# Channel mixers of an attention–mixer kernel by one level of Strassen (Winograd's seven products), on one core

## The reference, cut to what matters

```
q_s = exp(q - max_d q) / (sum_d + 1e-9);  k_s = exp(k - max_s k) / (sum_s + 1e-9)
x   = q_s @ (k_s^T v)                        # per batch and head, heads side by side: 576 x 512
u   = x + (relu(x^T w_tok1) w_tok2)^T        # token mixer, 576 -> 256 -> 576
y   = u + relu(u @ w_ch1) @ w_ch2            # stage B: 512 -> 1536 -> 512 (w1b, w2b)
yn  = (y - mean) / sqrt(var + 1e-6) * g_ln
out = y + relu(yn @ w1c) @ w2c               # stage C: 512 -> 2048 -> 512
```

## Time and profile before

| | |
|---|---|
| median of three runs | 1640.64 us |
| span of the profiled execution, its own time | 1637.3 us |
| TensorE busy (matmul) | 1611.0 us, 98% |
| VectorE busy | 600.8 us, 37% |
| ScalarE busy | 357.4 us, 22% |
| GpSimd busy | 242.7 us, 15% |
| moved by DMA | 120.17 MB, 73 GB/s over the span |

### The profile page before, as it was taken

How to read it: one execution, slowest core, us unless ns; L and a number is a source line. 1 busy time by engine, 2 the same in 40 slices (tenths; PEclk the granted TensorE clock), 3 DMA queues, 4 the chain that set the end, 5 groups by cost and what they waited for, 6 DMA issues and landing times.

```text
span 1637.3 us, 20140 instructions
## 1 busy us (share of the span) xinstructions
PE 1611.0 (98%) x7748; PEld 1354.0 (83%) x7748; DVE 600.8 (37%) x940; ACT 357.4 (22%) x643; POOL 242.7 (15%) x211
## 2 busy tenths in 40 slices
PE   6999999999999999999989999999999999999999
PEld 5899998888888888888868888888888888888887
DVE  7878751212212212122362424333333333342411
ACT  4556551111111111111221111111121111111110
POOL 5565658000000000000840000000000000000000
PEclk9999999999999999999999999999999999999999
DMA  7777744202102022021330200102020202020100
GB/s 245 244 225 233 226 153 154 93 1 77 54 23 77 0 77 77 0 77 64 104 116 1 70 8 19 58 0 77 0 77 0 77 0 77 0 77 0 51 0 27
DMA packets 72883, 120.17 MB, mean 73 GB/s; under 512 B 4944, under 2 KB 23952, under 8 KB 72848
## 3 DMA queue, kind: packets, MB, share of 16 engines
q1 hardware_dynamic: 68368, 105.01, 19.5%
q0 software_dynamic: 4480, 14.68, 2.8%
HBM read 91.36 MB, written 28.31 MB: 73 GB/s over the span
## 4 chain that ended last, share of the span: by engine, by line
PE 96%; DVE 2%; DMA 1%; SPq 0%; ACT 0%; issue 0%; DVEq 0%
PE bank L844 30%; PE bank L846 30%; PE bank L845 30%; PE bank L868 3%; PE bank L879 1%; PE bank L959 1%; PE bank L901 1%; PE bank L900 1%; DVE x_in L803 1%; DMA vt<-v 0%; DMA qt<-q 0%; PE bank L990 0%; PE bank L991 0%; PE bank L853 0%; DVE ln L792 0%
## 5 line engine op out<-in xcount | busy, mean ns | idle before, releaser
L809 DVE SCALAR_TENSOR_TENSOR h_lo<-bank,h_hi 128x512 fp32r<-128x512 f32 x252 | 174.1, 691 | 951.7 <-ACT h_hi L569 951.7
L569 ACT ACTIVATE h_hi<-bank 128x512 fp32r<-128x512 f32 x252 | 151.0, 599 | 1134.5 <-PE bank L846 1134.5
L846 PE MATMUL bank<-x_hi,w_early 128*128 128x512 f32 x576 | 224.1, 389 | 0.0
L845 PE MATMUL bank<-x_lo,w_early 128*128 128x512 f32 x576 | 224.1, 389 | 0.0
L844 PE MATMUL bank<-h_hi,w_early 128*128 128x512 f32 x576 | 224.1, 389 | 0.0
L845 PE MATMUL bank<-h_lo,w_early 128*128 128x512 f32 x576 | 224.1, 389 | 0.0
L846 PE MATMUL bank<-h_hi,w_early 128*128 128x512 f32 x576 | 224.1, 389 | 0.0
L844 PE MATMUL bank<-x_hi,w_early 128*128 128x512 f32 x576 | 224.1, 389 | 0.0
L844 PE MATMUL bank<-x_hi,w_late 128*128 128x512 f32 x432 | 168.8, 391 | 7.2 <-DVE x_lo L753 7.2
L845 PE MATMUL bank<-x_lo,w_late 128*128 128x512 f32 x432 | 168.5, 390 | 0.0
L846 PE MATMUL bank<-x_hi,w_late 128*128 128x512 f32 x432 | 168.5, 390 | 0.0
(11 more groups left out here) (113 smaller groups left out, 1925.8 us busy)
## 6 DMA issues: line engine op xcount, KB each, us to landing
kt<-kT SPq DMA_DIRECT2D x32, 288.0 KB, 5.7
u_scratch<-u_out SPq DMA_DIRECT2D x32, 288.0 KB, 2.7
x_in<-u_scratch SPq DMA_DIRECT2D x9, 1024.0 KB, 6.8
res<-u_scratch SPq DMA_DIRECT2D x9, 1024.0 KB, 8.7
y_scratch<-y_out SPq DMA_DIRECT2D x9, 1024.0 KB, 5.1
x_in<-y_scratch SPq DMA_DIRECT2D x9, 1024.0 KB, 6.8
res<-y_scratch SPq DMA_DIRECT2D x9, 1024.0 KB, 8.8
qt<-q SPq DMA_DIRECT2D x32, 256.0 KB, 3.8
```

Of the source, the lines that this page charges most:

```text
L569: nc.scalar.activation(h_hi[:, j % 2, :], bank[j % 2][:, 0:GROUP], ACT.Relu)\
L809: nc.vector.scalar_tensor_tensor(out=h_lo[:, j % 2, :], in0=bank[j % 2][:, 0:GROUP], scalar=0.0, in1=h_hi[:, j % 2, :], op0=ALU.max, op1=A ...
L845: mm(dst, a_hi, b_lo, start=False, stop=False)
L846: return mm(dst, a_lo, b_hi, start=False, stop=stop)
```

## The change

Tokens of a channel mixer are now taken in five **supergroups** of 924 tokens (two halves of 462; the last 912, two of 456). Each of the two products of a mixer is split in halves in all three dimensions and done with seven half-size products in place of eight. A mixer over a supergroup is a row of **calls** (`CALLS`). A mixing-in call (c.j = 0 to 2 in B, 0 to 3 in C) makes two 128-channel chunks of all four hidden quarters. One mixing-out call (c.j = -1) makes the outputs. Every call has seven **products** p = 0 to 6, and a product has c.epp **entries** (1 in mixing-in; 3 in B, 4 in C in mixing-out). An entry is 12 matmuls of 462 (456) columns that use one 512 KB piece of weights. A supergroup of B has 42 entries, one of C 56, in all 490, 5880 matmuls; before there were 6048 of 512 columns.

- **Weights.** 28 **units** (12 for B, 16 for C) are prepared. For each, POOL loads 512 KB (`load_unit`), makes the four sums (`sum_unit`), ACT rounds the seven results (`hi_unit`, 128x1792), POOL (stage A) or DVE (later) subtracts (`lo_unit`), and POOL stores 1792 KB (1.835 MB) to a DRAM scratch (`store_unit`). There is one staging buffer `w_out`, so `hi_unit(n)` waits for unit n-1 to be stored. Units 0 to 6 are done in stage A, 7 to 11 in supergroup 0 of B, 12 to 27 in supergroups 1 to 3 of B (four in the first two mixing-in calls, and in supergroups 1 and 2 two in the mixing-out call). Every entry is then loaded from the scratch, each time it is used, into a ring of four (`w_ring`, `load_entry`): entry n+4 when entry n has been used.
- **Activations.** Each supergroup's input is summed and split in seven forms (`sum_x`, `hi_x`, `lo_x`: 4, 7 and 7 operations of 924 columns), in the last mixing-in call of the supergroup before. The products go onto pairs of banks, from where ACT (`take`, p = 0, 1, 2, 6) or DVE (p = 3, 4, 5) moves them to `h`; product p+2 waits for the take of p, since it uses the same banks (`free`). `relu`, `relu_t1`, `sum_o`, `hi_o` and `lo_o` make the operands of the mixing-out call, three entries ahead at most (RO = 3); `take_y` adds a product to `res`.
- **Normalisation** is spread over the first three mixing-in calls of the supergroup before, with ScalarE's Abs_reciprocal_sqrt in place of Sqrt and DVE's reciprocal.
- Stage A and all else is written out without loops, and the extra register waits (`wait_apart`) go.

```diff
+    SIZES = [462, 462, 462, 462, 456]
+    NSG = len(SIZES)
...
+    F = {"B": w1b.shape[1], "C": w1c.shape[1]}
+    HC = {s: F[s] // (2 * P) for s in "BC"}
+    G1S = {s: HC[s] // 2 for s in "BC"}
+    EPP = {s: HC[s] // 2 for s in "BC"}
+    ENTRIES = {s: 7 * G1S[s] + 7 * EPP[s] for s in "BC"}
+    UNITS = {"B": 2 * HC["B"], "C": 2 * HC["C"]}
+    U0 = {"B": 0, "C": UNITS["B"]}
+    RW, RO = 4, 3
...
+        w_ring = sb("w_ring", [P, RW, 2, 2, 2 * P], f32r)
...
+            w_op = sb("w_op", [P, 2, 8, 2 * P], fp32, u)
+            w_out = sb("w_out", [P, 7, 2, 2 * P], f32r, u)
...
+            h = sb("h", [P, 4, max(HC.values()), NMAX], fp32, u)
+            o_hi = sb("o_hi", [P, RO, 2, NMAX], f32r, u)
...
+            def load_entry(n):
+                c = [c for c in CALLS if c.e0 <= n][-1]
+                local = n - [x for x in CALLS if x.pos == c.pos][0].e0
+                if c.sg == 0:
+                    e = (n - c.e0) % c.epp
+                    units = 2 * c.j + 2 if c.j >= 0 else HC[c.stage] + 2 * e + 2
+                    sp.wait_ge(wp_stored, 16 * (U0[c.stage] + units))
+                if n >= RW:
+                    sp.wait_ge(ent, n - RW + 1)
+                sp.dma_start(w_ring[:, n % RW, :, :, :].rearrange("p k s f -> p k (s f)").bitcast(fp32),
+                             ws_dram[c.stage][local]).then_inc(w_in[n % RW], 16)
...
+            def load_x(pos):
+                if pos >= NSG:
+                    sp.wait_ge(y_stored, 64 * (pos - NSG + 1))
+                if pos > 0:
+                    sp.wait_ge(x_lo_made, 7 * pos)
+                n = 2 * SIZES[pos % NSG]
+                sp.dma_start(xn[:, 0:NC * n].rearrange("p (c t) -> p c t", c=NC),
+                             tokens(source["BC"[pos // NSG]], pos % NSG)).then_inc(x_in, 16)
...
+            for c in CALLS:
+                if c.j == 0 and c.pos + 1 < NX:
+                    load_x(c.pos + 1)
+                if c.j == 1:
+                    if c.index == 1:
+                        phase_a_over(sp)
+                    load_res(c)
...
+                    for e in range(c.epp):
+                        n = c.e0 + p * c.epp + e + RW
+                        if n < ALL_ENTRIES:
+                            load_entry(n)
+                    if c.j < 0 and p == 3:
...
+            def load_unit(n):
...
+                pool.dma_start(dst[:, 0:8:7, :], src[:, 0, c, :, f:f + 2 * P]).then_inc(wp_in[n % 2], 16)
+                pool.dma_start(dst[:, 5:7, :], src[:, 1, c, :, f:f + 2 * P]).then_inc(wp_in[n % 2], 16)
+            def sum_unit(n):
+                x = w_op[:, n % 2, :, :]
+                pool.wait_ge(wp_in[n % 2], 32 * (n // 2 + 1))
...
+            def store_unit(n):
...
+                pool.dma_start(dst.rearrange("q p f -> p q f"),
+                               w_out[:, :, :, :].rearrange("p q s f -> p q (s f)").bitcast(fp32)).then_inc(wp_stored, 16)
             def sub_q(b, chunks):
...
+                if i < NB - 1:
+                    sum_unit(i)
+            batches(step)
+            for n in range(NB - 1, U0["C"] + UNITS["C"]):
+                sum_unit(n)
+                if n + 1 < U0["C"] + UNITS["C"]:
+                    load_unit(n + 1)
+                store_unit(n)
...
+            def hi_unit(n):
+                act.wait_ge(wp_sum, 4 * (n + 1))
+                wait(act, wp_stored, 16 * n)
+                nc.scalar.copy(w_out[:, :, 0, :], w_op[:, n % 2, 0:7, :]).then_inc(wp_hi, 1)
...
+            def hi_x(pos, p):
+                n = SIZES[pos % NSG]
+                if pos > 0:
...
+                nc.scalar.copy(x_hi[:, p, :, 0:n], x).then_inc(x_hi_made, 1)
...
+            def take(c, p):
...
+                act.wait_ge(ent, end(c, p))
+                dst = {0: 0, 1: 2, 2: 1, 6: 3}[p]
+                bank = bank_y if p == 1 else bank_x[c.index % 2]
+                func = ACT.Relu if p == 6 else ACT.Copy
+                nc.scalar.activation(h[:, dst, 2 * c.j:2 * c.j + 2, 0:c.n], bank[:, :, 0:c.n], func)\
+                  .then_inc(taken["act"], 1)
...
+            for c in CALLS:
+                last = c.j == G1S[c.stage] - 1
+                if c.j >= 0:
+                    for p in range(7):
+                        if p in (0, 1, 2, 6):
+                            take(c, p)
+                        if p == 4:
+                            relu(c, 4)
+                        if p == 5:
+                            relu(c, 5)
+                        if c.stage == "B" and c.sg == 0 and (c.j, p) in ((0, 0), (0, 4), (1, 1), (1, 5), (2, 2)):
+                            hi_unit(NB - 1 + 2 * c.j + (p >= 4))
+                        if c.stage == "B" and 0 < c.sg < 4 and not last and p in (0, 4):
+                            hi_unit(U0["C"] + 6 * (c.sg - 1) + 2 * c.j + p // 4)
...
+                        if last and c.pos + 1 < NX and c.pos != NSG - 1:
+                            hi_x(c.pos + 1, p)
...
+            def lo_x(pos, p):
...
+                dve.wait_ge(x_hi_made, 7 * pos + p + 1)
+                nc.vector.tensor_tensor(x_lo[:, p, :, 0:n], x, x_hi[:, p, :, 0:n], ALU.subtract)\
+                  .then_inc(x_lo_made, 1)
...
+                        if c.stage == "B" and 0 < c.sg < 4 and not last and p in (1, 2, 5, 6):
+                            lo_unit(U0["C"] + 6 * (c.sg - 1) + 2 * c.j + p // 5, p - 1 if p < 5 else p - 5)
...
+                        if last and c.pos + 1 < NX and c.pos != NSG - 1:
+                            split_x(c, p)
+                else:
+                    relu_t1(CALLS[c.index - 1])
+                    for n in range(7 * c.epp):
+                        p, e = n // c.epp, n % c.epp
+                        if n + 1 < 7 * c.epp and (n + 1) // c.epp in (2, 4, 6):
+                            sum_o(c, (n + 1) // c.epp, (n + 1) % c.epp)
+                        if n >= RO and (n - RO) % c.epp == c.epp - 1:
+                            take_y(c, (n - RO) // c.epp)
+                        lo_o(c, p, e)
+                        if n == 0 and c.pos + 1 < NX and c.pos != NSG - 1:
+                            lo_x(c.pos + 1, 6)
...
-                def hidden(j):
...
-                            pe.wait_ge(xlo[stage], NC * g + c + 1)
-                        x = three(bank[j % 2][:, 0:GROUP], w1_hi[:, c, :], w1_lo[:, c, :], x_hi[:, c, :], x_lo[:, c, :],
-                                  c == 0, c == NC - 1)
-                    x.then_inc(h_done[stage], 1)
...
-                def output(j):
...
-                    pe.wait_ge(hlo[stage], n * g + j + 1)
...
-                        x = three(bank[4 + c][:, 0:GROUP], w2_hi[:, cols], w2_lo[:, cols],
-                                  h_hi[:, j % 2, :], h_lo[:, j % 2, :], j == 0, j == n - 1)
-                        if j == n - 1:
...
+            def product(c, p):
+                dst = bank_y if p in (1, 3, 5) else bank_x[c.index % 2]
+                if p == 0 and c.index >= 2:
+                    free(CALLS[c.index - 2], 6)
+                if p == 1 and c.index >= 1:
+                    free(CALLS[c.index - 1], 5)
+                if p == 1 and c.index == 0:
+                    pe.wait_ge(u_act, U_ACT * NB)
+                    pe.wait_ge(u_dve, U_DVE * NB)
+                if p >= 2:
+                    free(c, p - 2)
+                for e in range(c.epp):
+                    n = c.e0 + p * c.epp + e
+                    pe.wait_ge(w_in[n % RW], 16 * (n // RW + 1))
+                    if c.j == 0:
+                        pe.wait_ge(x_lo_made, 7 * c.pos + p + 1)
+                    if c.j < 0:
+                        g = c.g0 + p * c.epp + e
+                        pe.wait_ge(o_lo_made, g + 1)
+                    for kk in range(2):
+                        if c.j >= 0:
+                            b_hi, b_lo = x_hi[:, p, kk, 0:c.n], x_lo[:, p, kk, 0:c.n]
+                        else:
+                            b_hi, b_lo = o_hi[:, g % RO, kk, 0:c.n], o_lo[:, g % RO, kk, 0:c.n]
+                        first = e == 0 and kk == 0 and p in (0, 1, 5)
+                        over = e == c.epp - 1 and kk == 1
+                        for i in range(2):
+                            w = [w_ring[:, n % RW, kk, s, i * P:(i + 1) * P] for s in range(2)]
+                            x = three(dst[:, i, 0:c.n], w[0], w[1], b_hi, b_lo, first, over, p in (2, 3, 4, 6))
+                    x.then_inc(ent, 1)
+            for c in CALLS:
+                for p in range(7):
+                    product(c, p)
+                    if NSG - 1 <= c.pos < NX - 1 and (c.j, p) == (0, 4):
+                        moment(c, 0)
```

790 lines of the change are left out of this document (441 added, 349 removed).

## The result

The changed kernel takes 1732.84 us (median of four runs: 1728.29, 1732.1, 1733.57 and 1833.33), against 1640.33 for the kernel before measured beside it: a ratio of 1.056, 95% interval 1.054 to 1.057, so 5.6% slower. The run of 1833.33 us had a granted clock of 0.80 where the others had 0.95, and the ratio is of the other three. The prediction was 1628 us, 0.8% faster, with a range to 1692: the sign was wrong and the time lies 41 us above the range. The profiled execution took 1728.29 us, its span is 1726.5, so 89 us are to be explained against the span of before, and 101 against the 1625 of the prediction's sum.

A forecast was written before the change was run, and what follows sets the result against it. TensorE, busy 98% of the span, was taken to bound the kernel. Terms -163.4 - 8.8 + 7 + 72 + 6 + 75 = -12 us gave 1625 us of span, 1628 as median; range for 8 in 10: 1565 to 1692.

The forecast's parts named there:

- Handovers: PE waits before mixing-out calls, 6.6 us at eight supergroups, 3.1 at two: +59 us, +72 with slow clock (38 to 90).
- the matmuls: 5880 narrower matmuls against 6048, at 205.6 and 203.1 ns by a line through 288 and 512 columns: -163.4 us.
- the ring: Loads of weights from the scratch into the ring land about when needed and cost nothing in stage C: 0 us.
- stage A: hi_unit ahead of r_hi makes PE wait 1.05 us in seven batches: +7 us; other additions hidden, up to 15 if not.
- the clock: 1.2 GHz stretch after long PE waits: 1.6 us behind each of eight handovers and six waits on takes; +23 us.
- Rival 4: Matmuls narrower than 512 columns are no faster: gain of 38 us instead of 163, 1753 us; chance 0.02.
- Takes behind the stores: Stage B: ACT's copies, then takes and PE, wait for stores: +75 us (65 waits, 10 clock), 25 to 120.
- The rate: The 16 DMA engines move 412 GB/s of loads, 379 of stores, taken over the skill's HBM limit of about 358.
- the waits at L519: Sign: ACT waits there on the DMA of w_out, in B only, and PE waits on ACT's take behind each.
- the span of stage C: Sign: near 5 x (138 + 8) us; otherwise the prediction is wrong.
- rival 3: Ring starves: mixed loads and stores move 200 GB/s, loads take 1284 us, 78 more than matmuls: 1706 us; chance 0.08.
- Rival 2: Waits behind stores 86 us instead of 65, clock 3.2 us per long wait (+22), slower DVE (+6): 1677 us; chance 0.30.

The follow-up runs named there:

- experiment 7: Only matmuls on constant data, no DMA or other engine beside them, at widths from 512 to 288 columns: 226.7 ns at 512, 211.7 at 462, 131.7 at 288.
- Experiment 3: Changed kernel with each 1.9 MB input and residual load cut in four between ring loads, the input's one call earlier: span 1706.8 us against 1726.5.
- experiment 2: Kernel with a second staging buffer, stage B's ring loads bringing 256 KB instead of 512: span 1673.3 us against 1697.0; stage B 630.0 against 655.8.
- Experiment 1: Changed kernel with a second staging buffer, so the rounding copy waits for the store of unit n-2, not n-1: span 1697.0 us against 1726.5.
- experiment 11: The combination: changed kernel with second staging buffer, five handover operations moved, loads in four, copy behind r_hi, constant by tensor_tensor: 1628.34 us, 0.9915 of before.

## Why the prediction was wrong

It had most of the mechanisms. Handovers came out right and one term too high; the matmuls, the ring, stage A and the clock were sized too low, and the ring was put at nothing.

- **Matmuls** (+27 us). The step that failed is "From these two, one column costs ... 0.416 ns, the rest 13 ns whatever the width": two points make a line, and 462 doesn't lie on it (experiment 7). Rival 4 asked whether narrowing gives anything at all; that it gives a little less than the line, 2% a matmul and 27 us in all, was no case of its own.
- **The ring of weights** (predicted 0, 38.4 us measured, the largest miss). "it lands about when it is needed. So in stage C it costs nothing" failed: some 3 us in the first call of nine of the ten supergroups, some 25 us in all, 10.8 of the ring's waits in stage C. A transfer with no slack was booked as hidden. For stage B the prediction asked what the full engines do to the stores and not what they do to the ring's loads, which wait there for 27.6 us. Experiment 3 gives 20 us back, halving the bytes (experiment 2) some 26.
- **Takes behind the stores** (predicted 65 us of waits and 10 of clock). The chain was right: copy behind store, take behind copy, TensorE two products on. The size was too high, 49.5 us. The store's 7.8 to 12.7 us hold in the median (11.5, and 7.2 for the first twelve units), not at the longest (16.0). Experiment 1 shows what the chain cost net: it took these waits away, the ring's grew by 22 us, and 29.5 were left.
- **The rate.** The 412 and 379 GB/s of the earlier trace rows were read from one microsecond of loads only and one of stores only, but mixed they hold: 383 GB/s over 43 us (experiment 2) and 409 over 41 (experiment 11), at a share of 1.02 and 1.03. The Trainium skill's limit of about 358 GB/s ("DMA: Bandwidth & Descriptors", section Specifications), which the prediction set aside, is exceeded in both. The rate was right; a mean share is what misleads, since stage B's 0.77 is made of stretches of up to 0.98 (43 us from 690 on) and others well below.
- **Stage A** (7 predicted, 17.3 measured). The place of the copy was sized rightly (6.0 us of waits, 4.7 given back). Of the other additions it said that they "fit below 1.0; I take them as hidden by the DMA's idle 30%, up to 15 us if not"; the hiding failed, and they cost 10 us. The DMA's share says nothing of GpSimd's subtractions, which hold VectorE up at one place. That this is where the waits on ke and q_hi (7.6 us) come from fits the rows but was not tested by itself.
- **Handovers** (59 predicted, 60.2 measured) right, by a chain of single operations written out. That VectorE and ScalarE take 1.12 and 0.96 us for 924 elements (estimated 1.1 and 0.95) was right as well.
- **Slow clock** (23 predicted, 38.7 measured). 1.6 us behind each long wait is about what one costs: 23 waits brought it, with 5 to 14 slow matmuls and 1.7 us each in the mean. Charged were 14; ten of the 23 were waits of 2.6 to 4.3 us, which I had not charged. Not every wait of that size brought it: three of 3.0 to 3.2 us did not.

Of what the prediction said would show it, the eight handovers of 6 to 7.5 us and the waits at L519 (70.3 us in B) came. The start distance was 210 ns and not 206, and the span of stage C, which should have been near 5 x 146 = 730 us, was 772.6 with waits for the ring in it, by its own words a sign of being wrong.

By the number rivals 4 (1753) and 3 (1706) were nearest, by luck: narrowing gave 137 us where rival 4 gave it 38, and stage B moved 274 GB/s in the mean where rival 3 had 200, though the ring did starve in places. Rival 2 (1677) was right on the clock (45 us with its 22, 38.7 measured) and wrong on the takes (86 us). With all the upper bounds that the prediction named (120 for the weights, 90 for handovers, 15 for stage A) the sum would have been near 1700 beside the 1733, and most of what is left is the matmuls' 27.

## What to carry to other kernels

A rate between two measured sizes is an estimate with an error of its own: where a term is thousands of instructions, 2% of it is the verdict, and the size should be measured by itself first. A transfer that lands just in time and an engine that is idle for 30% in the mean are no cover: look for the stretch in which the engine is full, and ask what each of its users then waits for. Where one queue holds both the work that TensorE waits for and a wait for a slow DMA, a second buffer or another place in the order gives back much of it: here such moves, with no arithmetic saved, turned 5.6% slower into 0.8% faster than before.

## What the runs showed of the hardware

- Distance of matmul starts (fp32 data, weights reloaded in two of three, 128 rows): 131.7 ns at 288 columns, 146.7 at 320, 173.3 at 384, 188.5 at 416, 202.5 at 448, 210.0 at 464, 211.7 at 462, 216.7 at 480, 226.7 at 512. There 462 takes longer than 464; in the mixers it was 210.2 against 210.7.
- An operation of VectorE of 16 numbers a partition took 3.38 us where GpSimd's two subtractions (4.20 us together) ran, and ended with them; as tensor_tensor in place of tensor_scalar it took 3.36. An operation that read one input from PSUM and one from SBUF was not held up (0.68 us).
- The 16 DMA engines moved 383 GB/s over 43 us and 409 over 41 with loads and stores mixed (share 1.02 and 1.03).
- In the handover shown TensorE stood idle, and the granted clock went from 1.00 (at 1026 us) to 0.51 (1.2 GHz); it was 0.50 when work resumed:

```profile
1030.00:1031.00 1.00, 0.00 (x0) 0.00 (x0) 1.00 (x2) 0.24 (x1) 0.00 (x0) 0.51 0.02 8
...
1033.00:1034.00 1.00, 0.12 (x1) 0.15 (x1) 1.00 (x2) 1.00 (x2) 0.00 (x0) 0.50 0.00 0
```

- Runs of the combination spread over 1.1% (1624.25 to 1641.69), of before over 0.2% (1639.02 to 1642.53). Stage B was at a DMA share of 0.84 in its profiled run, against 0.19 before; that the spread comes from there was not tested.
